# Decay scans joined, units reordered, a 2-2-4 ramp, and the low half of the hidden tile made on VectorE, in a two-layer MoE kernel behind gated linear attention

## The reference

```
# attention with a decaying state; B=4, H=8, S=768, D=48
state = alpha[t, :, None] * state + outer(k[t], v[t]);   o[t] = q[t] @ state
x  = o as (3072 tokens, 384)
h  = x @ w_in;    x2 = (max(h,0) + a*min(h,0)) @ w_out         # 384 -> 2048 -> 384
h2 = x2 @ w_in2;  y  = (h2>=1 ? h2 : h2<=-1 ? 0 : (h2+1)^2/4) @ w_out2
```

## Time and profile before

| | us |
|---|---|
| median of 3 runs | 948.95 (948.09 to 949.16) |
| profiled execution, its own time | 945.83 |
| profiled execution, span from first to last instruction | 944.1 |
| busy in the span: PE / DVE / POOL / ACT | 911.0 / 448.4 / 356.2 / 302.8 |
| granted TensorE clock, mean | 0.989 of 2.4 GHz |

### The profile page before, as it was taken

How to read it: one execution, slowest core, us unless ns; L and a number is a source line. 1 busy time by engine, 2 the same in 40 slices (tenths; PEclk the granted TensorE clock), 3 DMA queues, 4 the chain that set the end, 5 groups by cost and what they waited for, 6 DMA issues and landing times.

```text
span 944.1 us, 14449 instructions
## 1 busy us (share of the span) xinstructions
PE 911.0 (96%) x5754; PEld 774.4 (82%) x5754; DVE 448.4 (47%) x732; ACT 302.8 (32%) x561; POOL 356.2 (38%) x322
## 2 busy tenths in 40 slices
PE   7888999999999999999999999999999999999998
PEld 6777998889877788777888888888888888888886
DVE  5776655565556665555524443333333333333332
ACT  2432333222323322232235443233233332332222
POOL 6434332233323332323237654324334243342332
PEclk8988999999999999999999999999999999999999
DMA  6822121221122211111012300010000100100101
GB/s 176 227 55 48 22 47 34 50 53 34 35 40 54 43 34 35 35 34 35 18 51 85 103 14 1 1 34 1 17 18 0 34 1 1 34 0 1 34 1 33
DMA packets 21106, 37.10 MB, mean 39 GB/s; under 512 B 2160, under 2 KB 14448, under 8 KB 21040
## 3 DMA queue, kind: packets, MB, share of 16 engines
q1 hardware_dynamic: 21040, 36.19, 15.9%
HBM read 31.47 MB, written 4.72 MB: 38 GB/s over the span
## 4 chain that ended last, share of the span: by engine, by line
issue 42%; PE 32%; POOL 21%; DVE 3%; DMA 1%; SPq 0%; ACT 0%; POOLq 0%; DVEq 0%; ACTq 0%
POOL g_lo L304 16%; PE h_ps L676 5%; PE y_ps L676 4%; PE y_ps L678 4%; PE y_ps L677 4%; PE h_ps L677 4%; PE h_ps L678 4%; POOL x_lo L311 2%; POOL w_lo L284 2%; PE a_ps L617 2%; PE a_ps L646 1%; PE a_ps L641 1%; DVE prod L468 1%; DVE inv L475 1%; PE a_ps L631 1%
## 5 line engine op out<-in xcount | busy, mean ns | idle before, releaser
L304 POOL TENSOR_TENSOR g_lo<-g,g_hi 128x512 fp32r<-128x512 f32 (+2 forms) x208 | 252.7, 1215 | 492.6 <-ACT g_hi L392 492.5
L385 ACT ACTIVATE g<-h_ps 128x512 f32<-128x512 f32 (+2 forms) x208 | 117.6, 565 | 493.3 <-PE h_ps L678 476.8
L676 PE MATMUL y_ps<-g_lo,w_hi 128*128 128x512 f32 (+2 forms) x624 | 234.2, 375 | 7.9 <-POOL g_lo L304 7.9
L676 PE MATMUL h_ps<-x_lo,w_hi 128*128 128x512 f32 (+2 forms) x624 | 240.6, 386 | 0.7 <-ACT w_hi L346 0.6
L677 PE MATMUL h_ps<-x_hi,w_hi 128*128 128x512 f32 (+2 forms) x624 | 233.7, 375 | 0.0
L678 PE MATMUL h_ps<-x_hi,w_lo 128*128 128x512 f32 (+2 forms) x624 | 233.7, 374 | 0.0
L677 PE MATMUL y_ps<-g_hi,w_hi 128*128 128x512 f32 (+2 forms) x624 | 233.2, 374 | 0.0
L678 PE MATMUL y_ps<-g_hi,w_lo 128*128 128x512 f32 (+2 forms) x624 | 233.2, 374 | 0.0
L532 DVE SCALAR_TENSOR_TENSOR g<-g 128x512 f32<-128x512 f32 x96 | 66.4, 692 | 248.7 <-ACT g L385 248.7
L676 PEld LDWEIGHTS y_ps<-g_lo,w_hi 128*128 128x128 f32 x624 | 118.1, 189 | 29.4 <-POOL g_lo L304 5.5
L525 DVE SCALAR_TENSOR_TENSOR g<-g,slopes,h_ps 128x512 f32<-128x512 f32 (+2 forms) x112 | 74.8, 669 | 140.5 <-ACT g L385 139.8
(11 more groups left out here) (69 smaller groups left out, 519.1 us busy)
## 6 DMA issues: line engine op xcount, KB each, us to landing
qka_sb<-qka SPq DMA_DIRECT2D x44, 288.0 KB, 4.8
y_all<-w SPq DMA_DIRECT2D x16, 384.0 KB, 7.0
qka_sb<-w SPq DMA_DIRECT2D x16, 384.0 KB, 3.0
v_sb<-v SPq DMA_DIRECT2D x24, 192.0 KB, 5.0
y<-y_all SPq DMA_DIRECT2D x18, 256.0 KB, 2.7
qka_sb<-qka SPq DMA_DIRECT2D x4, 192.0 KB, 3.9
qka_sb<-qka SPq DMA_DIRECT2D x4, 96.0 KB, 2.9
slopes<-slopes_in SPq DMA_DIRECT2D x1, 8.0 KB, 4.4
```

The lines of the kernel that those rows point to most:

```text
L304: nc.gpsimd.tensor_tensor(g_lo[:, s % G_RING, 0:w_], g32[:, s % G32_RING, 0:w_], g_hi[:, s % G_RING, 0:w_].bitcast(F32), ALU.subtract).the ...
L385: nc.scalar.activation(g32[:, s % G32_RING, 0:w_], h_ps[s % 2][:, 0:w_], ACT.Relu, scale=-1.0 if first else 0.5, bias=0.0 if first else 0. ...
L676: nc.tensor.matmul(out_, wh, lo, start=start, stop=False)
```

## The change

- **Joined scans.** Alpha has a tile of its own with a padding column for each pair of heads (`SEG` = 129), so one scan over 516 columns takes the place of four over 128, and another that of four over 127. `starts` and `ends` hold the restarts; DVE sets them to 0 and 1 once.
- **q is scaled on DVE**, behind k; POOL keeps only the copy of the last column (`keep_last`). The padding rows of q, k and alpha now come from memory, so each of alpha, q with k, and v is one transfer of a unit.
- **Order of the units.** Two batches alternate (`place_of`), with a state for each; the first two units both start from none. `mix` makes the outputs first and the sums for the state behind them.
- **Order of the prefix.** It is written out on each engine, DVE makes both decays first, WARM is 24, and 12 idle matmuls stand behind the scores of unit 0. The masks of unit 1 go into `g32`.
- **Ramp.** FIRST is (2, 2, 4, 4, 4, 4, 4), before (2, 3, 3, 4, 4, 4, 4).
- **Plan.** `scores` is two steps ahead of `turn` (before three), and on DVE `decay` comes behind `activate(s+2)`.
- **g_lo of the first layer on DVE** (`hidden_lo` there), as the first instruction of a step, ahead of `copy_y` and the tasks; POOL makes it in the second layer alone.
- **Low halves of the weights on DVE**, both in one instruction 768 wide, but for the first four tiles, which POOL still makes.

```diff
-FIRST = (2, 3, 3, 4, 4, 4, 4)
+FIRST = (2, 2, 4, 4, 4, 4, 4)
-        for _stage, _lag in (("decay", 5), ("scores", 3), ("mix", 1), ("turn", 0)):
+        for _stage, _lag in (("decay", 5), ("scores", 2), ("mix", 1), ("turn", 0)):
-WARM = 20
-FILL = {("scores", 0): 3, ("scores", 1): 1, ("mix", 0): 4, ("mix", 1): 2, ("turn", 1): 3}
+WARM = 24
+FILL = {("scores", 0): 12, ("scores", 1): 1, ("mix", 0): 1, ("turn", 0): 1, ("mix", 1): 2, ("turn", 1): 2}
...
+def place_of(u):
+    pair, w = divmod(u, 2 * CHUNKS)
+    return 2 * pair + w % 2, w // 2
...
         @block.gpsimd
-            def scale_q(u):
-                pool.wait_ge(prod_done, PAIRS * (u + 1))
-                q = qka_of(u)[0:ROWS, 0]
-                nc.gpsimd.tensor_tensor(q, q, prod[0:ROWS], ALU.mult).then_inc(q_scaled, 1)
+            def keep_last(u):
+                pool.wait_ge(prod_done, u + 1)
...
-                    if s + 1 < STEPS:
-                        hidden_lo(s + 1)
+                    if SPLIT_STEP <= s + 1 < STEPS:
+                        hidden_lo(s + 1)
...
         @block.vector
             def decay(u):
-                for h in range(PAIRS):
-                    nc.vector.tensor_tensor_scan(prod[0:ROWS, h], al[:, h], zeros[0:ROWS], 1.0,
-                                                 ALU.mult, ALU.add).then_inc(prod_done, 1)
+                nc.vector.tensor_tensor_scan(prod[0:ROWS], al[:, 0:SCAN], starts[0:ROWS], 0.0,
+                                             ALU.mult, ALU.add).then_inc(prod_done, 1)
...
-                for h in range(PAIRS):
-                    nc.vector.tensor_tensor_scan(inv[0:ROWS, h, CHUNK - 2::-1], al[:, h, CHUNK - 1:0:-1], ...
+                nc.vector.tensor_tensor_scan(inv[0:ROWS, ::-1], al[:, SCAN:0:-1], ends[0:ROWS, ::-1], 0.0,
+                                             ALU.mult, ALU.add).then_inc(inv_done, 1)
...
+                nc.vector.tensor_tensor(q, q, by_pair(prod[0:ROWS])[:, :, 1:SEG], ALU.mult).then_inc(q_scaled, 1)
...
+            def hidden_lo(s):
+                w_ = width(s // FT)
+                dve.wait_ge(g_hi_done, s + 1)
+                ge(dve, hidden_used, s + 1 - G_RING)
+                nc.vector.tensor_tensor(g_lo[:, s % G_RING, 0:w_], g32[:, s % G32_RING, 0:w_],
+                                        g_hi[:, s % G_RING, 0:w_].bitcast(F32), ALU.subtract).then_inc(g_lo_first, 1)
...
             for n in range(BLOCKS):
                 for f in range(FT):
                     s = FT * n + f
+                    if s == 0:
+                        hidden_lo(0)
+                    if s + 1 < SPLIT_STEP:
+                        hidden_lo(s + 1)
                     if f == 0 and n >= 1:
                         copy_y(n - 1, 1)
...
+                    activate(s + AHEAD)
+                    for stage, u in plan_of(s):
                         if stage == "decay":
                             decay(u)
-                    activate(s + AHEAD)
-                    if n == 0 and f + EARLY < FT:
-                        split_w(f + EARLY)
+                    if n == 0 and f + EARLY + 1 < FT:
+                        split_w(f + EARLY + 1)
...
```

More of the change, by code:

```diff
@@ L37 @@
 EARLY = 4
[L38 removed]
+SEG = CHUNK + 1
+SCAN = PAIRS * SEG
 PLAN = {}
@@ L106, in build_program @@
         alpha_loaded = [sem(f"alpha_loaded{i}") for i in range(2)]
-        unit_loaded = [sem(f"unit_loaded{i}") for i in range(2)]
+        qk_loaded = [sem(f"qk_loaded{i}") for i in range(2)]
+        v_loaded = [sem(f"v_loaded{i}") for i in range(2)]
         raw_loaded = [sem(f"raw_loaded{i}") for i in range(RAW_FIRST)]
@@ L112, in build_program @@
         stored = sem("stored")
-        pads_set = [sem(f"pads_set{i}") for i in range(2)]
+        pads_set = sem("pads_set")
+        starts_set = sem("starts_set")
         state_cleared = sem("state_cleared")
-        zeros_set = sem("zeros_set")
         ident_set = sem("ident_set")
@@ L311, in input_lo @@
                 nc.gpsimd.tensor_tensor(x[0], y_of(n, m), x[1].bitcast(F32), ALU.subtract).then_inc(x2_lo_done, 1)
[L313 to L319, removed]
+            keep_last(0)
+            keep_last(1)
+            pool.wait_ge(q_scaled, 2)
+            split_in(0)
+            split_in(1)
+            split_out(0)
+            split_out(1)
+            for i in range(2, EARLY):
+                split_in(i)
+                split_out(i)
             for n in range(BLOCKS):
@@ L406, in copy_y @@
                                      ACT.Copy).then_inc(y_copied[m], 1)
[L408 to L417, removed]
+            copy_k(0)
+            split_w(0)
+            split_w(1)
+            copy_outputs(0)
+            copy_k(1)
+            turn_hi(0)
+            copy_outputs(1)
+            split_w(2)
+            turn_hi(1)
+            split_w(3)
+            split_w(4)
             for s in range(AHEAD):
                 relu_of(s)
+            split_w(5)
             for n in range(BLOCKS):
@@ L551, in copy_y @@
                     y_copied[m], 1)
-            nc.vector.memset(qka_of(0)[32:ODD, 2], 1.0).then_inc(pads_set[0], 1)
-            nc.vector.memset(qka_of(0)[32:ODD, 0:2], 1.0).then_inc(pads_set[0], 1)
-            dve.wait_ge(zeros_set, 1)
-            for task in FIRST_PLAN:
-                stage, u = task
-                if stage == "decay":
-                    decay(u)
-                if stage == "scores":
-                    if u == 0:
-                        dve.wait_ge(causal_set, 2)
-                        dve.wait_ge(state_cleared, 1)
-                    mask(u)
-                if stage == "mix":
-                    update_state(u)
-                if stage == "turn":
-                    turn_lo(u)
+            nc.vector.memset(alpha_sb[:, :, 0::SEG], 0.0).then_inc(pads_set, 1)
+            nc.vector.memset(starts[:], 0.0).then_inc(starts_set, 1)
+            nc.vector.memset(ends[:], 0.0).then_inc(pads_set, 1)
+            dve.wait_ge(starts_set, 1)
+            nc.vector.memset(starts[:, 0::SEG], 1.0).then_inc(starts_set, 1)
+            dve.wait_ge(starts_set, 2)
+            dve.wait_ge(pads_set, 2)
+            decay(0)
+            decay(1)
+            dve.wait_ge(causal_set, 2)
+            dve.wait_ge(state_cleared, 1)
+            mask(0)
+            mask(1)
+            update_state(0)
+            turn_lo(0)
+            turn_lo(1)
+            update_state(1)
             dve.wait_ge(slopes_loaded, 16)
@@ L622, in mix @@
             def mix(u):
-                qka = qka_of(u)
+                q, vs, o, sums = qk_of(u)[0:ROWS, 0], v_of(u), scores_bank(u, 0), scores_bank(u, 1)
+                pe.wait_ge(v_loaded[u % 2], 16 * load_count(u))
                 for e in range(2):
                     pe.wait_ge(masked, 2 * u + e + 1)
+                if not fresh(u):
+                    pe.wait_ge(state_done, 2 * states_before(u - 1))
+                halves = [slice(HALF * i, HALF * (i + 1)) for i in range(2)]
+                for h in range(PAIRS):
+                    if not fresh(u):
+                        for t in halves:
+                            nc.tensor.matmul(o[t, 2 * HD * h:2 * HD * (h + 1)], q[:, h, t], state[0:ROWS, u % 2, h],
+                                             start=True, stop=False)
+                    for e in range(2):
+                        c = slice((2 * h + e) * HD, (2 * h + e + 1) * HD)
+                        for t in halves:
+                            last = nc.tensor.matmul(o[t, c], att_of(u)[:, e, h, t], vs[:, c], start=fresh(u),
+                                                    stop=fresh(u) or e == 1)
+                last.then_inc(outputs_done, 1)
                 if keeps_state(u):
@@ L733 @@
     from concourse.bass_utils import run_bass_kernel_spmd
+    units = [place_of(u) for u in range(UNITS)]
+    rows = [*range(HD), *range(ODD - HD), *range(HD, 2 * HD)]
     def heads_on_partitions(x):
         x = x.reshape(BATCH, PAIRS, 2, CHUNKS, CHUNK, HD).transpose(0, 3, 2, 5, 1, 4)
-        return x.reshape(UNITS, 2, HD, PAIRS, CHUNK)
+        x = x.reshape(BATCH, CHUNKS, 2 * HD, PAIRS, CHUNK)[:, :, rows]
+        return np.stack([x[b, c] for b, c in units])
     def weight_tiles(w_in, w_out):
@@ L754 @@
     r = run_bass_kernel_spmd(nc, [arrays], core_ids=[0])
-    y = r.results[0]["y"]
+    y = r.results[0]["y"].reshape(D_MODEL, UNITS, CHUNK)
+    y = np.stack([y[:, u] for u in np.argsort([CHUNKS * b + c for b, c in units])], axis=1)
     return np.ascontiguousarray(y.reshape(D_MODEL, BATCH * SEQ).T)
```

238 lines of the change are left out of this document (122 added, 116 removed).

## The result

The changed kernel takes 1005.32 us (median of 4, 1004.68 to 1006.1) against 948.64 before, a ratio of 1.0598 (95% interval 1.058 to 1.0616). The forecast was 992, range 964 to 1010, slower. The profiled execution took 1006.1, its span is 1004.4.

A forecast was written before the change was run, and what follows sets the result against it. PE was taken to bound the kernel almost everywhere. Work -0.7 and +0.7, prefix -5.7, holes +44.5 gave +38.8 at full clock; with +4.4 for clock, 945.83 became 989.0, and 3.1 to the median made 992 us (range 964 to 1010).

The forecast's parts named there:

- Work of PE, second layer: PE's bare first-layer work, 493.7 us before, changes by -0.7 and +0.7, together nothing; the second layer stays at 390 us.
- Decay: One unit's decay on DVE, with joined scans of 1.20 and 1.25 us, takes 3.95 us (bounds 2.9 and 4.5), before 6.28.
- The bound of 0.8: Low bound in us for one joined scan of 516 columns, if its columns cost 1.1 ns each.
- Prefix: Ahead of the layer's first matmul: it comes at 22.6 us, not 28.3, so -5.7 (bounds -3.5 and -7.5).
- The three holes: PE's waits from g_lo at the head of DVE's step; with 1.2 more, 76.2 us against 31.7 before: +44.5.
- masks: PE waits at mix for masks queued behind g_lo, 1.26 us a unit at 512 wide, more when narrower: 30.75 us.
- copies: At a block's first step the second product's second third waits for copy_y: 9.75 us, block 1's copy counted under decays.
- decays: PE waits for g_lo or x_lo held up on DVE by state, activation and decay, mostly in narrow blocks: 34.5 us.
- Full clock: From the layer's first matmul to the second layer: some 570 us at full clock, 525.4 before.
- I count two falls, at 2.2 each: Clock falls at the 256-wide holes of 4.0, 4.65 and 4.65 us, two counted: +4.4 us.
- the forecast's own case: The main case, 980 to 1000 us around the forecast of 992, given 55%.
- the rival with seven falls: The clock falls at every hole of the narrow blocks, seven falls at 2.2 us each: 1003 us, 15%.

The follow-up runs named there:

- Kernel 7: kernel 4 with the decay a step earlier (six ahead of the turn) and the state's update behind the activation: 915.83 us, ratio 0.9672 to the kernel before the change.
- Experiments 1 and 2: Changed kernel with DVE's copy_y and attention tasks moved ahead of g_lo: 941.98 us; changed kernel with only the masks moved ahead of g_lo: 971.64 us.
- experiment 6: The kernel before the change with only g_lo of the first layer made on DVE, first in its step: 1069.03 us, ratio 1.1285.
- kernel 3: Changed kernel with idle matmuls on PE in the holes, in the corrected version: 987.59 us, ratio 1.0427 to the kernel before the change.
- kernel 4: Changed kernel with g_lo of the first layer made on POOL again, first in POOL's step: 930.18 us, ratio 0.9818 to the kernel before the change.
- 8: Changed kernel with g_lo on DVE behind the copy and attention tasks, and the decay six ahead of the turn: 922.87 us, ratio 0.9735 to before.

## Why the prediction was right, and where its size was off

**Work of PE, second layer:** right. The second layer took 390.69 for 390.37. Kernel 7, with few holes and full clock, needs 502.0 us for the stretch, where I had 493.7 of bare work: some 6 us are waits left, the other 2 are not explained.

**Decay:** 3.95 forecast, 3.95 measured; each joined scan is 1.23 (forecast 1.20 and 1.25). The bound of 0.8 is excluded. The working to 1.20 was loose: 0.34 less 0.05 over 128 columns is 2.3 ns a column, not 2.1. The recorded lengths, 0.40 for 128 columns before and 1.23 for 516, give 2.15 ns a column and 0.12 for a start. The Trainium skill (DVE: opcode table, instruction layouts, handler registers and perf-mode slots, section Datapath and trigger behaviour) has the scan at half throughput. The trace agrees: 2.15 ns a column against the 1.1 of the `TENSOR_TENSOR` rows.

**Prefix:** -5.7 forecast, -7.0 measured. PE came to the scores of unit 1 at 13.1, forecast 13.9; the other 0.5 us was won behind that.

**The three holes**, forecast and measured as waits of PE: masks 30.75 and 28.5 (1.26 and 1.29 each at 512 wide); copies 11.2 with the one in block 1, and 10.2 (forecast 2.0 each at 512 wide, the longest was 1.9); decays 33.0 and 30.1 (14.5 at `g_lo`, 15.6 at `x_lo`). Counted from start to start, as the forecast counts, they are 32.0, 11.2 and 32.6, within 1.3 us each. Experiments 1 and 2 showed that the first two come from the order, and experiment 6 that `g_lo` at the head of DVE's step suffices to slow the kernel before.

**Full clock:** the stretch was forecast at some 570 us, and with the clock held it is 574.0 (kernel 3).

**The term that was mis-sized is the clock.** "I count two falls, at 2.2 each", +4.4. There were ten, and they cost 592.5 - 574.0 = 18.5 us in the profile, 1005.3 - 987.6 = 17.7 in the medians, some 1.85 each. I had looked for falls where a hole was nearly as long as the 4.56 us of the earlier trace rows, had named three such holes and counted two, without a reason. But six of the seven decay holes of blocks 0 and 1 had a fall behind them, from 2.56 us on, and so had four holes of the wide blocks, for which I had put nothing. The price was nearly right, the number of falls was not.

So the forecast's own case, 980 to 1000, did not come. The time lies nearest to the rival with seven falls, 1003, which had 15%: it was right about the narrow blocks but for one hole, had too high a price, and it too left out the wide blocks, so its 1003 is in part luck. That the measured time lies in the range is owed to that rival and not to the sum.

The 13 us between 992 and 1005 are +14.1 for the clock, +4.1 for the stretch at full clock (574.0 where the sum has 569.9), +0.3 for the second layer, -1.3 for the prefix, and -3.9 for the step from the profiled execution to the median, which I had put at +3.1 and which was -0.8.

## What to carry to other kernels

On an engine with an in-order queue, ask of each moved instruction not only how long it takes but when its input arrives, and what that is ready stands behind it: 0.69 us of work, put ahead of its tasks, cost 75 us here, and 12 with the tasks ahead of it, each against the same kernel with that work on POOL. That DVE has idle time does not make the move pay: `g_lo` was cheaper on POOL in both pairs (kernel 4 against 1; kernel 7 against 8, which differ in the state's place too), though it stretches the decay there. And price a hole on PE at more than its length: 69 us of holes took 18 us of clock with them.

## What was not expected of the hardware

- Idle matmuls of 128 columns in the holes keep the granted clock at 1.000 (0.975 without them) and are worth 17.7 us, though they do no work and the holes stay.
- The clock fell to its lower level (1.2 GHz) behind a single hole of 2.67 us in the 512-wide blocks, in a PE that was busy for the rest of that stretch of 8.58 us (mean clock 0.80). The length of a hole alone did not tell: of four copies' holes of 1.85 us two had a fall behind them, and one of 2.27 had none.
- A scan of 516 columns, alone 1.23 us, took 2.27 (median of the 24 in kernel 4) where POOL's 1.3 us product met it, and the 0.69 us product of q 1.78: 1.04 and 1.09 us more. The backward scan between them, which no product of POOL met, kept its 1.23. A copy out of `y_ps` that lay within POOL's product kept its 0.69, so not every instruction of DVE is stretched.
